# Windowed attention with two gated convolutions: turned probabilities in three blocks of 128 columns instead of four

## The chip, the cores and the metric

The program runs on one core of a Trainium2 chip. A core has TensorE (matmuls, PE in the profile, its weight loads PEld), VectorE (DVE), ScalarE (ACT), GpSimd (POOL) and SyncE (SP, which here issues all the DMAs). The metric is the device time of one execution in microseconds (us). The kernel before took 472.19 us, the median of three runs (470.36 to 472.33).

## The reference

The input is q, k and v of 4 batches, 8 heads, 576 positions, 64 per head. A query sees itself and the 127 keys before it, with a slope of its own for each head:

```
scores = q k^T / 8 ; mask = (0 <= i-j < 128)
scores = where(mask, scores - slope[h]*|i-j|, -1e9)
attn   = exp(scores - max) / (sum + 1e-9) ; x = attn v     # (4, 576, 512)
h = relu(x @ w_in)                                         # 512 -> 1024
conv_out = sum over 3 taps of conv_w[k] * h[s + k - 1]
x = (h * sigmoid(conv_out)) @ w_out                        # 1024 -> 512
gate = sigmoid(sum over 5 taps of conv_w2[k] * x[s + k - 4])
y = (gate * (x @ w_val)) @ w_out2                          # 512 -> 512
```

Everything is float32. The change touches only the product `attn v`.

## The kernel before, in words

**Attention in steps.** One step is one query tile `t` of 128 positions (five tiles to a sequence: 0 to 4, the last, `FULL`, has 64) and one pair of heads `hp`. There are 20 steps to a batch and 80 in all: 16 with t=0, 48 with t=1 to 3 (called full steps here), 16 with t=4. A tile is cut in two halves of 64 queries. The scores of one half are a matrix of 128 rows (64 queries of one head, then 64 of the other) by 192 keys: the queries of a half see the 128 keys before its first and its own 64. `scores` on PE (L732) makes them, DVE adds the bias and finds the maximum (L519), ACT takes the exponential and the sum (L388), DVE divides (L551).

**Turn and mix.** PE then turns the probabilities with the identity (`turn`, L746) so that keys lie on the partitions, ACT copies the turned ones from PSUM to `probs_t` (L399), and `mix` (L767) multiplies them with the values into `o_ps`. `probs` holds a half in 256 columns, of which 192 are used and 64 are zero, so that a block of 128 columns is always one whole key tile: a full step has two halves and two key tiles, so four blocks. `mix` goes over the key tiles `j`, the one before and the own one, and over the two heads; one matmul takes the 64 queries of both halves of that head, 128 columns, and its 64 output rows are the head's dimensions. So a full step has 4 matmuls of 128 columns, a step of t=0 has 2 of 128 columns (its own key tile alone), a step of t=4 has 4 of 64 columns (one half; its own key tile has 64 keys, so these matmuls use 64 rows of the array). The two heads write to different halves of the output partitions.

**A float32 matmul in the profile.** Turns have one record each; scores and mixes have two records for each matmul (288 matmuls of L767 and 576 records). "128*64" in a row is the part of the array in use: 128 rows (keys) by 64 columns (a head's dimensions).

**Products.** The four dense layers are `product` (L786 to L788): each block is three matmuls of 288 or 290 columns. They are worked in 8 chunks `c` of 288 positions, in 24 beats `j` each (`up`, `val`, `down`, `out`).

**The order.** It is written out by hand in `walk`. The first 12 steps run alone (`run`), the other 8 of the first batch run alone in the middle of chunk 0, and the other 60 stand one to a beat among the `down` products (12 matmuls to a beat): `slot` (turn of this step, scores three steps ahead), then the products of the beat, then `close`, the mix. Chunks 2, 4, 6 hold the 8 steps of t=3 and 4, chunks 1, 3, 5 the 12 of t=0 to 2. Engines meet at counting semaphores (`wait_ge`, `reach`): `probs_normal` (DVE has divided), `turned`, `copied` (ACT has copied), `mixed`.

## Time and profile before

| | |
|---|---|
| median of the runs | 472.19 us |
| time of the profiled execution | 472.24 us |
| its span (first to last instruction) | 470.5 us |
| PE busy, records | 444.9 us (95%), 3424 |
| PE weight loads busy | 413.7 us (88%) |
| DVE busy | 319.6 us (68%) |
| ACT busy | 283.0 us (60%) |
| mean granted clock of TensorE | 0.989 |

A row of a group of instructions names line, engine, operation, output and inputs, shapes and the number of records. PE records overlap, since matmuls are pipelined: how fast PE works is read from the distance of their starts, not from the mean duration. Of TensorE's clock, 1.00 is 2.4 GHz and 0.50 is 1.2 GHz.

### The profile page before, as it was taken

To read this page: it belongs to the slowest core of one execution; us is meant where nothing else is said; L and a number is where in the kernel's file an instruction comes from. 1 tells how busy PE (TensorE), PEld (TensorE's weight loads), DVE (VectorE), ACT (ScalarE), POOL (GpSimd) and SP (SyncE) were. 2 spreads that over 40 slices of the span, in tenths; PEclk is the share of its full clock that TensorE was granted. 3 is DMA by queue.
4 is the path that set the end of the run, shared out by engine and by line. 5 is a ranking of instruction groups with operands and counts; after the bars stand their busy time and mean duration, and the time that the engine had idled before them with its cause. 6 is when DMAs were issued, how large, how long until landed. Compare 5 with 4: busy or idle time off the path is not lost.

```text
span 470.5 us, 9646 instructions
## 1 busy us (share of the span) xinstructions
PE 444.9 (95%) x3424; PEld 413.7 (88%) x3424; DVE 319.6 (68%) x1128; ACT 283.0 (60%) x788; POOL 82.1 (17%) x116
## 2 busy tenths in 40 slices
PE   4888589988999999999999999999999999999996
PEld 3668559987999998999989999999989998899995
DVE  6695897866874777477675767757777576847741
ACT  3576942577556864497546874398555875287131
POOL 3210991071000410022000220013000230014000
PEclk9999869999999999999999999999999999999999
DMA  8765112001211012111211012011211100010011
GB/s 195 211 208 228 45 36 57 0 13 34 68 47 62 2 46 69 39 37 45 70 46 38 26 47 66 26 50 47 68 37 35 38 1 0 11 43 2 0 52 50
DMA packets 38927, 25.80 MB, mean 55 GB/s; under 512 B 22752, under 2 KB 35040, under 8 KB 38880
## 3 DMA queue, kind: packets, MB, share of 16 engines
q1 hardware_dynamic: 38880, 25.20, 18.7%
q8 instruction: 27, 0.44, 0.4%
q14 instruction: 20, 0.16, 0.1%
HBM read 20.47 MB, written 4.72 MB: 54 GB/s over the span
## 4 chain that ended last, share of the span: by engine, by line
PE 82%; DVE 7%; ACT 5%; issue 2%; DMA 1%; POOL 1%; SPq 1%; ACTq 0%; DVEq 0%
PE bank L786 20%; PE bank L787 20%; PE bank L788 20%; PE bank L732 8%; PE bank L767 7%; PE bank L746 7%; DMA k_all<-k_t 1%; DVE probs L551 1%; DVE probs L519 1%; ACT conv L426 1%; DVE w_lo L574 1%; DVE conv L604 1%; DVE gate L660 1%; ACT conv L432 1%; ACT bank L417 1%
## 5 line engine op out<-in xcount | busy, mean ns | idle before, releaser
L786 PE MATMUL bank<-g_hi,w_hi 128*128 128x288 f32 x384 | 120.8, 315 | 1.6 <-DVE g_lo L634 1.6
L786 PE MATMUL bank<-x_hi,w_hi 128*128 128x290 f32 (+1 forms) x384 | 114.5, 298 | 2.8 <-DVE x_lo L594 1.4
L787 PE MATMUL bank<-x_lo,w_hi 128*128 128x290 f32 (+1 forms) x384 | 114.0, 297 | 0.0
L788 PE MATMUL bank<-x_hi,w_lo 128*128 128x290 f32 (+1 forms) x384 | 113.7, 296 | 0.0
L787 PE MATMUL bank<-g_lo,w_hi 128*128 128x288 f32 x384 | 113.3, 295 | 0.0
L788 PE MATMUL bank<-g_hi,w_lo 128*128 128x288 f32 x384 | 113.3, 295 | 0.0
L357 POOL TENSOR_TENSOR g_lo<-conv,g_hi 128x288 fp32r<-128x288 f32 x64 | 51.9, 812 | 331.4 <-ACT g_hi L440 331.4
L604 DVE SCALAR_TENSOR_TENSOR conv<-bank,taps,conv 128x288 f32<-128x288 f32 (+1 forms) x128 | 65.5, 513 | 54.2 <-ACT conv L426 53.9
L388 ACT ACTIVATE probs<-probs,neg_max 128x192 f32<-128x192 f32 (+2 forms) x144 | 62.0, 432 | 33.1 <-DVE neg_max L519 31.6
L786 PEld LDWEIGHTS bank<-x_hi,w_hi 128*128 128x128 f32 x384 | 72.5, 189 | 3.5 <-DVE conv L612 1.8
L786 PEld LDWEIGHTS bank<-g_hi,w_hi 128*128 128x128 f32 x384 | 72.2, 188 | 2.6 <-issue 2.3
L788 PEld LDWEIGHTS bank<-x_hi,w_lo 128*128 128x128 f32 x384 | 72.7, 189 | 0.0
L787 PEld LDWEIGHTS bank<-x_lo,w_hi 128*128 128x128 f32 x384 | 72.5, 189 | 0.0
L787 PEld LDWEIGHTS bank<-g_lo,w_hi 128*128 128x128 f32 x384 | 72.2, 188 | 0.0
L788 PEld LDWEIGHTS bank<-g_hi,w_lo 128*128 128x128 f32 x384 | 72.2, 188 | 0.0
L399 ACT COPY probs_t<-bank 128x512 f32<-128x512 f32 (+1 forms) x80 | 39.9, 499 | 50.3 <-PE bank L746 49.8
L732 PE MATMUL bank<-k_all,q_tile 128*128 128x192 f32 (+2 forms) x288 | 61.5, 337 | 6.6 <-DMA k_all<-k_t 6.6
L660 DVE SCALAR_TENSOR_TENSOR gate<-bank,taps,gate 128x288 f32<-128x288 f32 (+4 forms) x128 | 65.3, 510 | 2.6
L746 PE MATMUL bank<-identity,probs 128*128 128x128 f32 x256 | 47.4, 300 | 9.2 <-DVE probs L551 9.0
L732 PEld LDWEIGHTS bank<-k_all,q_tile 128*128 128x128 f32 x288 | 47.3, 207 | 7.0 <-issue 5.7
L767 PE MATMUL bank<-probs_t,v_tile 128*64 128x128 f32 (+2 forms) x576 | 49.5, 284 | 2.7 <-ACT probs_t L399 1.4
L519 DVE CUSTOM_DVE_ANT_0 probs<-bank,bias 128x192 f32<-128x192 f32 (+2 forms) x144 | 46.2, 326 | 2.9 <-PE bank L732 2.5
(44 smaller groups left out, 519.0 us busy)
## 6 DMA issues: line engine op xcount, KB each, us to landing
w_raw<-panels SPq DMA_DIRECT2D x12, 512.0 KB, 6.1
y_t<-y_sb SPq DMA_DIRECT2D x32, 144.0 KB, 1.8
q_tile<-q_t SPq DMA_DIRECT2D x32, 128.0 KB, 3.1
k_all<-k_t SPq DMA_DIRECT2D x16, 256.0 KB, 3.6
v_tile<-v_tiles SPq DMA_DIRECT2D x16, 256.0 KB, 2.7
q_tile<-q_t SPq DMA_DIRECT2D x8, 64.0 KB, 2.4
k_all<-k_t SPq DMA_DIRECT2D x4, 128.0 KB, 2.7
v_tile<-v_tiles SPq DMA_DIRECT2D x4, 128.0 KB, 3.9
```

The source lines that it names most:

```text
L357: pool.tensor_tensor(g1_lo[:, m, :], conv[n % DEPTH][:, :], g1_hi[:, m, :], ALU.subtract).then_inc(g1_lo_done, 1)
L388: last = act.activation(probs[r][:, half, lo:hi], probs[r][:, half, lo:hi], ACT.Exp, bias=neg_max[r][:, half:half + 1], scale=-1.0, accum_ ...
L399: act.copy(probs_t[step % 2][:, 0:cols], t_ps[:, 0:cols]).then_inc(copied, 1)
L519: ins = dve.tensor_tensor_reduce(probs[r][:, half, lo:hi], s_ps[step % 2][:, 2 * P * half + lo:2 * P * half + hi], bias_of(hp, t, half), - ...
L604: dve.scalar_tensor_tensor(out=out, in0=banks[UP_BANK[m]][:, at + skip_first:at + HALF - skip_last], scalar=taps1[:, tap, m:m + 1], in1=ou ...
L660: dve.scalar_tensor_tensor(out=out, in0=banks[m][:, tap + skip:tap + HALF], scalar=taps2[:, tap, m:m + 1], in1=out, op0=ALU.mult, op1=ALU. ...
L732: last = pe.matmul(s_ps[step % 2][:, 2 * P * half + lo:2 * P * half + hi], q_tile[tile % 2][:, hp, half, :, :], k_all[:, hp, first_key + l ...
L746: last = pe.transpose(t_ps[:, at:at + P], probs[step % RING][:, half, col:col + P], identity[:, :])
L767: last = pe.matmul(o_ps[rows, P * hp:P * hp + SUB * subs], v_tile[key_tile % V_RING][0:keys, P * hp + HEAD * h:P * hp + HEAD * (h + 1)], t ...
L786: pe.matmul(out, w_hi[:, p, col:col + P], hi(k), start=start, stop=False)
L787: pe.matmul(out, w_hi[:, p, col:col + P], lo(k), start=False, stop=False)
L788: last = pe.matmul(out, w_lo[:, p, col:col + P], hi(k), start=False, stop=stop)
```

## The change

`probs` of a full step becomes 384 columns without a gap: half 0 in columns 0 to 191, half 1 in columns 192 to 383 (`packed`). Three blocks are turned instead of four (`blocks_of`). Block 0 is half 0 against the tile before, block 2 is half 1 against the own tile, and block 1 holds both rests: in its first 64 turned rows half 0 against the first 64 keys of the own tile, in its last 64 half 1 against the last 64 keys of the tile before. ACT copies 384 columns instead of 512. `mix` becomes up to four parts (`part`), each a pair of matmuls, one to a head, with the 64 queries of one half: own keys 0 to 63 (block 1), the tile before (block 0), own tile (block 2), keys 64 to 127 of the tile before (block 1). The last part first waits for the first (`upper_mixed`). A step of t=0 has the first and the third part and still two blocks; t=4 has the first and second part, with the same matmuls as before in another order. DVE clears 4 stretches of zeros at the start instead of 8.

```diff
--- before.py
+++ after.py
@@ -98,12 +98,12 @@
         v_tile = [place(f"v_tile{s}", [P, MODEL]) for s in range(V_RING)]
         bias = place("bias", [P, PAIRS, SEEN])
         identity = place("identity", [P, P])
-        probs = [place(f"probs{r}", [P, 2, 2 * P]) for r in range(RING)]
+        probs = [place(f"probs{r}", [P, 3 * P]) for r in range(RING)]
         neg_max = [place(f"neg_max{r}", [P, 2]) for r in range(RING)]
         total = [place(f"total{r}", [P, 2]) for r in range(RING)]
         guarded = [place(f"guarded{r}", [P, 2]) for r in range(RING)]
         inverse = [place(f"inverse{r}", [P, 2]) for r in range(RING)]
-        probs_t = [place(f"probs_t{r}", [P, 4 * P]) for r in range(2)]
+        probs_t = [place(f"probs_t{r}", [P, 3 * P]) for r in range(2)]
 
         g1_hi = place("g1_hi", [P, KW, HALF], F32R)
         g1_lo = place("g1_lo", [P, KW, HALF], F32R)
@@ -144,6 +144,7 @@
         turned = sem("turned")
         copied = sem("copied")
         mixed = sem("mixed")
+        upper_mixed = sem("upper_mixed")
         x_hi_done = sem("x_hi_done")
         x_lo_done = sem("x_lo_done")
         up_done = sem("up_done")
@@ -191,6 +192,16 @@
             lo, hi = columns_of(t, half)
             return bias[:, hp, lo - SUB * half:SEEN]
 
+        def packed(t, half):
+            lo, hi = columns_of(t, half)
+            return P * half + lo, P * half + hi
+        def blocks_of(t):
+            return {0: (1, 2), FULL: (0, 1)}.get(t, (0, 1, 2))
         def width_of(t):
             return TAIL if t == FULL else P
 
@@ -384,19 +395,19 @@
                 r = step % RING
                 act.wait_ge(scores_kept, step + 1)
                 for half in halves_of(t):
-                    lo, hi = columns_of(t, half)
-                    last = act.activation(probs[r][:, half, lo:hi], probs[r][:, half, lo:hi], ACT.Exp,
+                    lo, hi = packed(t, half)
+                    last = act.activation(probs[r][:, lo:hi], probs[r][:, lo:hi], ACT.Exp,
                                           bias=neg_max[r][:, half:half + 1], scale=-1.0,
                                           accum_out=total[r][:, half:half + 1])
                 last.then_inc(probs_done, 1)
 
             def slot(step):
                 _, t, _ = where(step)
-                cols = 2 * P if t in (0, FULL) else 4 * P
+                lo, hi = P * blocks_of(t)[0], P * blocks_of(t)[-1] + P
                 act.wait_ge(turned, step + 1)
 
                 reach(act, mixed, step - 1)
-                act.copy(probs_t[step % 2][:, 0:cols], t_ps[:, 0:cols]).then_inc(copied, 1)
+                act.copy(probs_t[step % 2][:, lo:hi], t_ps[:, lo:hi]).then_inc(copied, 1)
                 if step + LOOK - 1 < ALL_STEPS:
                     exps(step + LOOK - 1)
 
@@ -493,8 +504,7 @@
                 dve.memset(q_tile[s][HEAD:P, :, :, 0, :], 0.0).then_inc(q_zeroed, 1)
                 dve.memset(q_tile[s][0:HEAD, :, :, 1, :], 0.0).then_inc(q_zeroed, 1)
             for r in range(RING):
-                dve.memset(probs[r][:, 0, SEEN:2 * P], 0.0).then_inc(probs_zeroed, 1)
-                dve.memset(probs[r][:, 1, 0:SUB], 0.0).then_inc(probs_zeroed, 1)
+                dve.memset(probs[r][:, SEEN:2 * P], 0.0).then_inc(probs_zeroed, 1)
 
             def make_bias(hp):
                 for h in range(2):
@@ -515,9 +525,9 @@
 
                     reach(dve, turned, step - RING + 1)
                     dve.wait_ge(scores_done, step + 1)
-                lo, hi = columns_of(t, half)
+                (lo, hi), (to, end) = columns_of(t, half), packed(t, half)
                 ins = dve.tensor_tensor_reduce(
-                    probs[r][:, half, lo:hi], s_ps[step % 2][:, 2 * P * half + lo:2 * P * half + hi],
+                    probs[r][:, to:end], s_ps[step % 2][:, 2 * P * half + lo:2 * P * half + hi],
                     bias_of(hp, t, half), -SCALE, 3e38, ALU.add, ALU.min,
                     neg_max[r][:, half:half + 1])
                 if half == halves_of(t)[-1]:
@@ -547,8 +557,8 @@
                     return
                 if half == 0:
                     dve.wait_ge(inverse_done, step + 1)
-                lo, hi = columns_of(t, half)
-                ins = dve.tensor_scalar(probs[r][:, half, lo:hi], probs[r][:, half, lo:hi],
+                lo, hi = packed(t, half)
+                ins = dve.tensor_scalar(probs[r][:, lo:hi], probs[r][:, lo:hi],
                                         inverse[r][:, half:half + 1], None, ALU.mult)
                 if half == halves_of(t)[-1]:
                     ins.then_inc(probs_normal, 1)
@@ -738,13 +748,9 @@
                 _, t, _ = where(step)
                 pe.wait_ge(probs_normal, step + 1)
                 reach(pe, copied, step)
-                blocks = 1 if t == 0 else 2
-                for half in halves_of(t):
-                    for j in range(blocks):
-                        at = (blocks * half + j) * P
-                        col = (2 - blocks + j) * P
-                        last = pe.transpose(t_ps[:, at:at + P], probs[step % RING][:, half, col:col + P],
-                                            identity[:, :])
+                for n in blocks_of(t):
+                    last = pe.transpose(t_ps[:, P * n:P * n + P], probs[step % RING][:, P * n:P * n + P],
+                                        identity[:, :])
                 last.then_inc(turned, 1)
 
             def mix(step):
@@ -755,19 +761,32 @@
 
                     reach(pe, x_lo_done, tile)
                 pe.wait_ge(copied, step + 1)
-                blocks = 1 if t == 0 else 2
-                subs = len(halves_of(t))
-                turned_probs = probs_t[step % 2][:, 0:subs * blocks * P].rearrange(
-                    "p (a j h i) -> p a j h i", a=subs, j=blocks, h=2)
-                for j in range(blocks):
-                    key_tile = tile - blocks + 1 + j
-                    keys = width_of(t) if j == blocks - 1 else P
+                own, prev = v_tile[tile % V_RING], v_tile[(tile - 1) % V_RING]
+                def part(half, n, values, keys, start, stop):
                     for h in range(2):
-                        rows = slice(HEAD * h, HEAD * h + HEAD)
-                        last = pe.matmul(o_ps[rows, P * hp:P * hp + SUB * subs],
-                                         v_tile[key_tile % V_RING][0:keys, P * hp + HEAD * h:P * hp + HEAD * (h + 1)],
-                                         turned_probs[0:keys, :, j, h, :], start=(j == 0),
-                                         stop=(j == blocks - 1))
+                        at = P * hp + SUB * half
+                        heads = P * hp + HEAD * h
+                        last = pe.matmul(o_ps[HEAD * h:HEAD * h + HEAD, at:at + SUB],
+                                         values[keys, heads:heads + HEAD],
+                                         probs_t[step % 2][keys, P * n + SUB * h:P * n + SUB * h + SUB],
+                                         start=start, stop=stop)
+                    return last
+                reach(pe, mixed, step)
+                last = part(0, 1, own, slice(0, SUB), True, t == 0)
+                if 0 < t < FULL:
+                    last.then_inc(upper_mixed, 1)
+                if t > 0:
+                    last = part(0, 0, prev, slice(0, P), False, True)
+                if t < FULL:
+                    last = part(1, 2, own, slice(0, P), True, t == 0)
+                if 0 < t < FULL:
+                    pe.wait_ge(upper_mixed, step // STEPS * PAIRS * (FULL - 1) + step % STEPS - PAIRS + 1)
+                    last = part(1, 1, prev, slice(SUB, P), False, True)
                 last.then_inc(mixed, 1)
 
             def slot(step):
@@ -891,7 +910,7 @@
             for step in range(LOOK):
                 scores(step)
             pe.wait_ge(identity_made, 1)
-            pe.wait_ge(probs_zeroed, 2 * RING)
+            pe.wait_ge(probs_zeroed, RING)
             walk(slot, mix, beat)
 
 
```

On PE, a full step among the `down` products of chunk 1, before: the mix of the step, the turn and the scores of the next beat (v_tile_61 is the tile before, v_tile_59 the own one).

```order
L767 MATMUL bank<-probs_t_85,v_tile_61 64x128 [waits copied]
L767 MATMUL bank<-probs_t_85,v_tile_61 64x128
L767 MATMUL bank<-probs_t_85,v_tile_59 64x128 x2
L746 MATMUL bank<-identity,probs_66 128x128 [waits copied,probs_normal]
L746 MATMUL bank<-identity,probs_66 128x128 x3
L732 MATMUL bank<-k_all,q_tile_57 128x192 [waits scores_kept]
L732 MATMUL bank<-k_all,q_tile_57 128x192
```

The same place now. A row `64x64` is 64 output rows by 64 columns.

```order
L771 MATMUL bank<-probs_t_85,v_tile_59 64x64 [waits mixed,copied]
L771 MATMUL bank<-probs_t_85,v_tile_59 64x64
L771 MATMUL bank<-probs_t_85,v_tile_61 64x64 x2
L771 MATMUL bank<-probs_t_85,v_tile_59 64x64 x2
L771 MATMUL bank<-probs_t_85,v_tile_61 64x64 [waits upper_mixed]
L771 MATMUL bank<-probs_t_85,v_tile_61 64x64
L752 MATMUL bank<-identity,probs_66 128x128 [waits copied,probs_normal]
L752 MATMUL bank<-identity,probs_66 128x128 x2
L742 MATMUL bank<-k_all,q_tile_57 128x192 [waits scores_kept]
L742 MATMUL bank<-k_all,q_tile_57 128x192
```

Four matmuls of 128 columns have become eight of 64 in four parts, the first and the last on 64 keys; one turn of four has gone, and each mix waits for the mix before it and once for its own first part.

On PE, a step of t=0 in chunk 1, before:

```order
L767 MATMUL bank<-probs_t_84,v_tile_61 64x128 [waits copied,x_lo_done,v_loaded2]
L767 MATMUL bank<-probs_t_84,v_tile_61 64x128
L746 MATMUL bank<-identity,probs_65 128x128 [waits copied,probs_normal]
L746 MATMUL bank<-identity,probs_65 128x128
L732 MATMUL bank<-k_all,q_tile_56 128x192 [waits scores_kept,qk_loaded0]
L732 MATMUL bank<-k_all,q_tile_56 128x192
```

The same place now:

```order
L771 MATMUL bank<-probs_t_84,v_tile_61 64x64 [waits copied,mixed,x_lo_done,v_loaded2]
L771 MATMUL bank<-probs_t_84,v_tile_61 64x64 x3
L752 MATMUL bank<-identity,probs_65 128x128 [waits copied,probs_normal]
L752 MATMUL bank<-identity,probs_65 128x128
L742 MATMUL bank<-k_all,q_tile_56 128x192 [waits scores_kept,qk_loaded0]
L742 MATMUL bank<-k_all,q_tile_56 128x192
```

Two matmuls of 128 columns have become four of 64, of which the first two use 64 keys; the turns are as many as before.

## Rows read from the trace of the kernel before

**Rows 1.** Page, section 1: busy time, share of the span, instructions of each engine.
```profile
PE 444.9 (95%) x3424; PEld 413.7 (88%) x3424; DVE 319.6 (68%) x1128; ACT 283.0 (60%) x788; POOL 82.1 (17%) x116
```
**Rows 2.** Page, section 4: the chain that ended last, by engine.
```profile
PE 82%; DVE 7%; ACT 5%; issue 2%; DMA 1%; POOL 1%; SPq 1%; ACTq 0%; DVEq 0%
```
**Rows 3.** Stretches: length, busy time (records) of each engine, PE clock, DMA.
```profile
12.20:19.10 6.90, 6.90 (x29) 4.95 (x30) 4.00 (x18) 2.94 (x13) 2.34 (x4) 1.00 1.09 282
19.10:37.30 18.20, 15.28 (x132) 11.65 (x132) 16.89 (x78) 13.77 (x43) 2.37 (x4) 1.00 0.61 197
56.00:73.80 17.80, 14.22 (x104) 10.42 (x104) 17.23 (x57) 10.41 (x33) 15.53 (x20) 0.71 0.19 53
80.00:470.50 390.50, 383.12 (x2992) 362.35 (x2990) 257.98 (x894) 236.21 (x647) 49.36 (x62) 1.00 0.13 37
```
**Rows 4.** Waits of PE and PEld from 80 us: total us, times, longest.
```profile
PEld bank L767 <- issue: 11.3, 60, 1.6
...
PE bank L786 <- DVE g_lo L634: 1.6, 1, 1.6
PE bank L767 <- ACT probs_t L399: 1.4, 1, 1.4
PE bank L786 <- DVE conv L612: 1.3, 1, 1.3
```
**Rows 5.** PE in order of time, t=0: start, length, line, x records.
```profile
114.39 0.44 PE L767 MATMUL bank<-probs_t,v_tile 128*64 128x128 f32 x4
114.76 0.44 PE L746 MATMUL bank<-identity,probs 128*128 128x128 f32 x2
```
**Rows 6.** PE in order of time, full step among products.
```profile
120.57 0.66 PE L767 MATMUL bank<-probs_t,v_tile 128*64 128x128 f32 x8
121.16 0.66 PE L746 MATMUL bank<-identity,probs 128*128 128x128 f32 x4
121.65 0.82 PE L732 MATMUL bank<-k_all,q_tile 128*128 128x192 f32 x4
```
**Rows 7.** PE in order of time, two full mixes with nothing between.
```profile
35.55 1.09 PE L767 MATMUL bank<-probs_t,v_tile 128*64 128x128 f32 x16
```
**Rows 8.** PE in order of time, t=4 among products (the x8 are both forms).
```profile
182.79 0.60 PE L767 MATMUL bank<-probs_t,v_tile 128*64 128x64 f32 x8
183.31 0.44 PE L746 MATMUL bank<-identity,probs 128*128 128x128 f32 x2
183.59 0.33 PE L732 MATMUL bank<-k_all,q_tile 128*128 128x64 f32 x2
```
**Rows 9.** The same t=4 mix, its second form alone.
```profile
183.05 0.33 PE L767 MATMUL bank<-probs_t,v_tile 64*64 64x64 f32 x4
```
**Rows 10.** PE in order of time, two t=4 mixes with nothing between.
```profile
72.77 1.12 PE L767 MATMUL bank<-probs_t,v_tile 128*64 128x64 f32 x16
```
**Rows 11.** The t=4 mix cut at 182.79 and at 182.895 us: records begun till then.
```profile
182.79 0.27 PE L767 MATMUL bank<-probs_t,v_tile 128*64 128x64 f32 x1
...
182.79 0.33 PE L767 MATMUL bank<-probs_t,v_tile 128*64 128x64 f32 x3
```
**Rows 12.** Instructions of L767 from 80 us on: their count and forms.
```profile
L767 PE MATMUL bank<-probs_t,v_tile x432: 218/273/324, 108.4 to 408.0; 128*64 128x128 f32 x114, 128*64 128x64 f32 x15, 64*64 64x64 f32 x15
```
**Rows 13.** ACT's copies of turned probabilities: busy, mean ns, idle before.
```profile
L399 ACT COPY probs_t<-bank 128x512 f32<-128x512 f32 x48 | 28.1, 585 | 30.5 <-PE bank L746 30.1
L399 ACT COPY probs_t<-bank 128x256 f32<-128x256 f32 x32 | 11.8, 370 | 19.8 <-PE bank L746 19.7
```
**Rows 14.** Two pieces of the chain, first run of steps: start, length, what.
```profile
23.57 0.66 PE bank L746 x4
...
24.88 0.59 PE bank L767 x8
```
**Rows 15.** PE in order of time, second run of steps, clock at 0.50.
```profile
57.09 1.12 PE L746 MATMUL bank<-identity,probs 128*128 128x128 f32 x4 [4.86 <-DVE probs L551]
...
63.96 1.11 PE L746 MATMUL bank<-identity,probs 128*128 128x128 f32 x4 [0.27 <-DVE probs L551]
```


## The prediction

> **What bounds the kernel now.** I read the page's busy times and its chain of waits first, then the stretches, then the waits of PE, and last PE's instructions in order of time. PE is busy for 95% of the span and its weight loads for 88%, against 68% for the next engine [rows 1], and PE makes up 82% of the chain that ended last [rows 2]. The reader is to see that both say the same: what PE does is the time. The stretches say where this doesn't hold. From 80 us to the end PE is busy 383.12 of 390.50 us, while DVE has 258 and ACT 236 [rows 3], and PE's waits there for another engine come to 1.6 + 1.4 + 1.3 = 4.3 us [rows 4]. The 60 steps that stand among products lie in that part (432 records of L767 are 36 full steps of 8, 12 steps of t=0 of 4 and 12 of t=4 of 8 [rows 12]). In the first run of steps PE is busy 6.90 of 6.90 us while the steps of t=0 pass, and 15.28 of 18.20 us in the full ones; in the second run of steps it is DVE that has no room, 17.23 of 17.80 us, with PE at 14.22 [rows 3].
>
> **How PE's time in a mix is made up.** Record lengths mislead, since matmuls overlap; the distances of starts don't. Two full mixes with nothing between take 1.09 us as one group where one takes 0.66 [rows 6, 7], so eight more records cost 0.43 us. The two heads start together (three records have begun by 182.895 us, of which two are one pair [rows 11]), so this is four pairs of 128 columns at 0.11 us. A full mix runs from 120.57 to 121.16, 0.59 us [rows 6]: four pairs are 0.44, and 0.15 are left over. A mix of t=0, two pairs, runs from 114.39 to 114.76, 0.37 us [rows 5]: 0.22 and again 0.15. The rest doesn't grow with the pairs: it is the price of changing the part of the array in use (128*128 to 128*64 and back), once for each block of matmuls with one part. The row that decides is that of t=4. Its mix has two such blocks, 128*64 and then 64*64; the first begins at 182.79, the second at 183.05, the turn at 183.31 [rows 8, 9]. Each block takes 0.26 us for two pairs of 64 columns. Two mixes of t=4 back to back cost 1.12 against 0.60 [rows 8, 10]: 0.52 more for two more blocks. A pair of 64 columns is half of 0.11, 0.055, so each block is 0.11 for its pairs and 0.15 for the change. So a change of the rows alone, at the same 64 columns, costs as much as a change from 128*128. The Trainium skill says so too ("TensorEngine Tiling (Array Packing)", Tiling Modes, Key Properties: changing the tiling mode, not just the tile, drains TensorE); by that rule, and the trace agrees in the one direction it has, 128 rows to 64, the direction from 64 rows to 128 drains as well, which no row here shows.
>
> **The change part by part.**
>
> *Full step, mix.* Four parts: 64*64, then 128*64 twice, then 64*64. That is three blocks and eight pairs of 64 columns: 3 x 0.15 + 8 x 0.055 = 0.89 us against 0.59, so +0.30. The columns that pass through the array are the same as before; all that is added is two changes of the part in use. The change from 64*64 to 128*64 stands in no row. From below it is free, as the change within one form is [rows 7], from above it is the 0.15 of rows 8 and 9. I take 0.15, the nearest row: the same two forms, the other way round.
>
> *Full step, turn.* Four turns take 0.49 us (121.16 to 121.65 [rows 6]), two take 0.28 (183.31 to 183.59 [rows 8]): 0.11 for one that goes. Net +0.19 us for a full step. The Trainium skill gives some 0.275 us for a transpose of 128x128 in a kernel ("TensorE: Matmul & The Clock Gate", Part 4: PE-mode transpose). The trace has 0.11 at a granted clock of 1.00 and decides; by the page's figure the 36 full steps would gain 5.9 us more, an estimate of about 476 for the whole.
>
> *Step of t=0.* Two blocks and four pairs of 64: 0.30 + 0.22 = 0.52 against 0.37, +0.15. Turns as before. *Step of t=4.* The same two blocks in the other order: 0.
>
> *The new waits.* The fourth part waits for the first part's end. It could start 0.26 + 0.15 + 0.22 = 0.63 us after the first began; the first is over after 0.26 plus a tail: the last form's group reads 0.33 from 183.05 [rows 9]. So it is met 0.3 us early, and what is queued behind it (the last pair of parts, then the next turn) isn't held. The wait of a mix for the mix before is met a whole beat earlier. Taken at 0; were each to cost 0.05, it would be 36 x 0.05 = 1.8 us.
>
> *ACT's copy.* 512 columns take 585 ns, 256 take 370 [rows 13], so 384 take some 478, 0.11 less. Among products it was over long before the mix (PE waits once for it, 1.4 us [rows 4]): 0 there.
>
> *DVE.* The same instructions on the same columns, four clears fewer, which lie beside the first load. 0.
>
> **The sum.** From 80 us on, where PE has nothing to wait for, all of it is exposed: 36 x 0.19 = 6.8 and 12 x 0.15 = 1.8, 8.6 us. First run: three mixes of t=0 fall in the stretch in which PE is never idle, +0.45. Its eight full steps: if the old chain held, it has six turns of x4, two mixes of x8 and two copies (a turn and a mix of them in [rows 14]): 2 x 0.30 - 6 x 0.11 - 2 x 0.11 = -0.3. If PE's work set the pace, 8 x 0.19 = +1.5; PE has 2.9 us free there [rows 3]. I take +0.5. Second run: four full steps under DVE's cover (PE has 3.6 us free [rows 3]), I take +0.05, bounds -0.1 and +0.8. Sum 9.6 us. Against the profiled execution's own 472.24 us (span 470.5 and 1.7 around it) this gives 481.8. The median of the runs is 472.19, so it needs no shift.
>
> **Rivals.**
> 1. *The change from 64 rows to 128 is free.* Then a full step has two dear changes and gives +0.15 - 0.11 = +0.04, t=0 gives 0: 36 x 0.04 = 1.5 us and nothing at the start, 473.9, no change to be measured. For it: no row shows this direction. Against it: the other one costs 0.15, and so do the ones to and from 128*128.
> 2. *Faster: rows can be changed without a stop when the 64 columns stay.* The place is inside each mix, and the price -0.11 us for each full step: 36 x -0.11 = -4.0, with -0.3 in the first run, 467.9. It decides from the point where such a change costs less than 36 x 0.11 / (2 x 36 + 12) = 0.047 us. Against it stands 182.79 to 183.05 for two pairs that need 0.11 [rows 8, 9].
> 3. *It is the number of records that costs.* The t=4 mix has 0.53 us for 8 records, 0.066 each; if that were a rate of issue, 16 records would take 1.06 and a full step +0.47 - 0.11 = +0.36: 36 x 0.36 + 12 x 0.16 + about 1.6 at the start is 16.5, 488.7. Against it: three records have begun within 0.11 us [rows 11], and 128-column records pass at 0.43 / 8 = 0.054 [rows 6, 7]. For it: nowhere do more than four records of 64 columns follow each other in one form. The Trainium skill has such a rate, some 62 ns for each MATMUL when the sequencer decodes in microcode ("TensorE: Matmul & The Clock Gate", Part 2: What happens when you issue a matmul); the row of 0.054 lies under it.
> 4. *The clock falls in the first run of steps.* It fell to 0.50 around 56 us, after PE had been idle for 4.86 us [rows 15]; the first run has no such gap, but its mixes get emptier. Cold steps take (63.96 - 57.09) / 2 = 3.4 us [rows 15] against 18.2 / 8 = 2.3 [rows 3]: some +9, 491.
>
> **How the numbers follow.** Forecast 0.79, rival 1 0.05, rival 2 0.05, rival 3 0.08, rival 4 0.03. The forecast's own range is 479 to 484.5: below, the first run at its lower bound and part of the row change hidden; above, the new waits at 0.05 each and the first run fully exposed. The range given, 478.5 to 489, takes in rival 3 and leaves out 1, 2, 4 and some tails, under 2 in 10. A change of 0.5%, 2.4 us, is about what can be told from none. Slower by over that: 0.79 + 0.08 + 0.03, less 0.01 for a forecast that fails in part, 0.89; within it 0.05; faster 0.06.
>
> **What would show it.** In the profile after, a full mix among products should run from its first start to the next turn in 0.89 us, with three blocks: 64*64 of 4 records (0.26), 128*64 of 8 (0.37), 64*64 of 4 (0.26). The full turn should go from 0.49 to 0.38, the mix of t=0 from 0.37 to 0.52, the beat of a full step grows by 0.19. The copies should read some 478 ns, the weight loads of L767's successor should show more idle time put down to issue than the 11.3 us of 60 times [rows 4], and the stretch of the second run should be as long as before. If the middle block starts within 0.15 us of the first, rival 1 or 2 is right; if the four pairs of the middle block take more than 0.25 us between their starts, rival 3. A row in which the fourth part waits for the first would show that the new wait isn't hidden.

## The result, and the profile after

The changed kernel takes 487.38 us, the median of four runs (485.66 to 490.24), against 471.27 before: a ratio of 1.0345 (95% interval 1.0311 to 1.0379), so 16 us slower. The forecast was 481.8 in a range of 478.5 to 489.0, chance of slower 0.89. The direction and, for the 60 steps among products, the mechanism were right, the size was not: 9.6 us forecast, some 16 measured. The profiled execution took 490.24 us, span 488.5, and is the slowest of the four; its lengths are read here, and the whole by the ratios. Medians below are of all runs of a kernel, while the ratios leave out three runs that lie over 1.5% above their kernel's fastest: one of 848.95 us in experiment 2, and 492.64 and 491.92 us in experiment 4.

From the page after: busy time, share and records of the engines, and the granted clock of TensorE in 40 slices, as in [rows 1].

```profile
PE 466.2 (95%) x3824; PEld 432.5 (89%) x3824; DVE 318.7 (65%) x1124; ACT 277.5 (57%) x788; POOL 82.3 (17%) x116
...
PEclk9998955999999999999999999999999999999999
...
PE 84%; DVE 5%; ACT 5%; issue 2%; DMA 1%; POOL 1%; SPq 1%; ACTq 0%; DVEq 0%
```

PE has 21 us more of busy time and is as full as before. What differs is the granted clock: in the sixth and seventh slice, 61 to 86 us, it is at 0.50, its lower level of 1.2 GHz, where before it was there for some 10 us, and the 8 in the fourth slice is a shorter low stretch (mean over the span 0.972, before 0.989).

PE among the products in the changed kernel, in order of time: start, length, group, records. First a step of t=0, then a full one; a group carries the form of its first record. They answer to [rows 5] and [rows 6].

```profile
124.31 0.60 PE L771 MATMUL bank<-probs_t,v_tile 64*64 64x64 f32 x8
124.84 0.33 PE L752 MATMUL bank<-identity,probs 128*128 128x128 f32 x1
...
134.32 0.97 PE L771 MATMUL bank<-probs_t,v_tile 64*64 64x64 f32 x16
135.22 0.55 PE L752 MATMUL bank<-identity,probs 128*128 128x128 f32 x3
135.60 0.33 PE L742 MATMUL bank<-k_all,q_tile 128*128 128x192 f32 x1
```

The mix of t=0 runs from 124.31 to 124.84, 0.53 us (forecast 0.52, before 0.37). The full mix runs from 134.32 to 135.22, 0.90 us (forecast 0.89, before 0.59), in blocks of 0.26, 0.38 and 0.26 by the starts of its single records, and the turn from 135.22 to 135.60, 0.38 (forecast 0.38, before 0.49). The rest of what was forecast is there too: ACT's copies, and PE's waits from 80 us on, which answer to [rows 13] and [rows 4].

```profile
L410 ACT COPY probs_t<-bank 128x384 f32<-128x384 f32 x48 | 23.0, 479 | 36.3 <-PE bank L752 36.1
```

```profile
PEld bank L771 <- issue: 12.0, 62, 1.7
...
PE bank L805 <- DVE g_lo L644: 1.6, 1, 1.6
PE bank L771 <- ACT probs_t L410: 1.5, 1, 1.5
PE bank L805 <- DVE conv L622: 1.3, 1, 1.3
...
PE bank L771 <- PE bank L771: 0.2, 1, 0.2
```

The last of these rows is one group of records, the last mix of the second run of steps:

```profile
81.08 0.89 PE L771 MATMUL bank<-probs_t,v_tile 64*64 64x64 f32 x8 [0.16 <-PE bank L771]
```

A copy takes 479 ns, and PE waits for other engines as little as before. The 0.16 us is a mix of t=4, which has no fourth part: it waits for the mix just before it, and the same happens where the last two mixes of the first run follow each other. The wait of a mix's fourth part for its first stands in no row, so it is hidden. One sign that was named hardly came: the idle of the weight loads put down to issue is 12.0 us here after 11.3. The new pauses inside a mix are hardly listed as waits; they are seen in the distances of starts.

What was not forecast is the first batch. Stretches of the changed kernel: length, busy time (records) of PE, PEld, DVE, ACT, POOL, then the clock. They are the first run of steps, the first products behind it, the second run, the first products behind that, and from the first mix among products to the last.

```profile
12.00:38.00 26.00, 25.15 (x204) 19.35 (x204) 19.09 (x89) 14.68 (x52) 5.03 (x8) 1.00 0.64 188
...
41.00:44.30 3.30, 3.01 (x12) 3.01 (x13) 0.24 (x1) 0.00 (x0) 0.00 (x0) 0.50 0.99 375
...
61.70:82.00 20.30, 19.58 (x134) 14.53 (x134) 16.10 (x57) 9.01 (x33) 14.14 (x18) 0.50 0.16 40
...
82.00:85.30 3.30, 3.30 (x14) 3.30 (x15) 0.42 (x1) 0.37 (x1) 0.00 (x0) 0.50 0.27 79
...
118.00:428.00 310.00, 309.71 (x2683) 289.41 (x2684) 205.59 (x770) 188.43 (x539) 32.72 (x41) 1.00 0.14 38
```

In the second run it was DVE that had no room, 17.23 of 17.80 us, with PE at 14.22 [rows 3]. Now PE has 19.58 of 20.30 and DVE 16.10: the bound has changed hands. The 18.0 us between the two profiled executions can be laid out by the starts of PE's instructions:

| stretch | before | now | more |
|---|---|---|---|
| start to the first product | 38.1 us | 41.3 us | 3.2 |
| from there to the first turn behind it | 12.9 | 14.6 | 1.6 |
| that turn to the next one (PE mostly waits for DVE) | 6.1 | 5.9 | -0.2 |
| the second run from there, to the first product behind it | 16.7 | 20.2 | 3.4 |
| from there to the first mix among products | 34.5 | 36.2 | 1.6 |
| to the end | 362.1 | 370.4 | 8.3 |

The last line is the one that the forecast had. The two of 1.6 us are the products that pass at the low clock, and the 3.4 lie in the second run. The first line is in part chance. Four records of the same scores, at the start and later, in the changed kernel and then in the one before:

```profile
17.65 1.49 PE L742 MATMUL bank<-k_all,q_tile 128*128 128x192 f32 x4
...
25.83 0.82 PE L742 MATMUL bank<-k_all,q_tile 128*128 128x192 f32 x4
```

```profile
14.89 1.49 PE L732 MATMUL bank<-k_all,q_tile 128*128 128x192 f32 x4
...
21.12 0.82 PE L732 MATMUL bank<-k_all,q_tile 128*128 128x192 f32 x4
```

At the start they follow each other at 0.32 us, later at 0.16, though the column of the granted clock reads 1.00 for both. The change comes at 23.9 us in the changed kernel's profile and at 18.4 in the one before; in the fourteen profiles of this case it lies between 13.1 and 23.9 us. The same changed kernel profiled again (experiment 3) has it at 19.7 and its first product 2.2 us earlier.

### The profile page after: what moved, and what is told of

Its sections match the earlier page's. It is cut to its first block, busy times and chain, and to the rows that moved or that the text cites. A ratio compares the mean times of both kernels' runs of the same rounds, so it can differ in the third digit from the quotient of the medians.

```text
span 488.5 us, 10521 instructions
## 1 busy us (share of the span) xinstructions
PE 466.2 (95%) x3824; PEld 432.5 (89%) x3824; DVE 318.7 (65%) x1124; ACT 277.5 (57%) x788; POOL 82.3 (17%) x116
## 4 chain that ended last, share of the span: by engine, by line
PE 84%; DVE 5%; ACT 5%; issue 2%; DMA 1%; POOL 1%; SPq 1%; ACTq 0%; DVEq 0%
PE bank L805 19%; PE bank L806 19%; PE bank L807 19%; PE bank L771 12%; PE bank L742 8%; PE bank L752 6%; DMA k_all<-k_t 1%; ACT conv L437 1%; DVE probs L561 1%; DVE probs L529 1%; DVE conv L614 1%; DVE gate L670 1%; ACT conv L443 1%; ACT bank L428 1%; ACT g_hi L451 1%
## 5 line engine op out<-in xcount | busy, mean ns | idle before, releaser
L771 PEld LDWEIGHTS bank<-probs_t,v_tile 128*64 128x64 f32 (+1 forms) x1024 | 49.5, 142 | 27.9 <-issue 16.0
L771 PE MATMUL bank<-probs_t,v_tile 128*64 128x64 f32 (+1 forms) x1024 | 70.4, 252 | 2.4 <-ACT probs_t L410 1.5
L742 PE MATMUL bank<-k_all,q_tile 128*128 128x192 f32 (+2 forms) x288 | 64.3, 348 | 6.4 <-DMA k_all<-k_t 6.4
L410 ACT COPY probs_t<-bank 128x384 f32<-128x384 f32 (+1 forms) x80 | 34.9, 436 | 60.2 <-PE bank L752 60.0
L742 PEld LDWEIGHTS bank<-k_all,q_tile 128*128 128x128 f32 x288 | 49.7, 217 | 6.9 <-issue 5.5
L752 PE MATMUL bank<-identity,probs 128*128 128x128 f32 x208 | 43.5, 314 | 6.3 <-DVE probs L561 6.0
```

The source lines that it names most:

```text
L410: act.copy(probs_t[step % 2][:, lo:hi], t_ps[:, lo:hi]).then_inc(copied, 1)
L742: last = pe.matmul(s_ps[step % 2][:, 2 * P * half + lo:2 * P * half + hi], q_tile[tile % 2][:, hp, half, :, :], k_all[:, hp, first_key + l ...
L752: last = pe.transpose(t_ps[:, P * n:P * n + P], probs[step % RING][:, P * n:P * n + P], identity[:, :])
L771: last = pe.matmul(o_ps[HEAD * h:HEAD * h + HEAD, at:at + SUB], values[keys, heads:heads + HEAD], probs_t[step % 2][keys, P * n + SUB * h: ...
```

## Experiments

Each kernel ran beside the kernel before, on one chip within a group; "us" is the median, the ratio that to the kernel before.

**1. All parts on 128 rows.**

```diff
-last = part(0, 1, own, slice(0, SUB), True, t == 0)
+last = part(0, 1, own, slice(0, SUB if t == FULL else P), True, t == 0)
-last = part(1, 1, prev, slice(SUB, P), False, True)
+last = part(1, 1, prev, slice(0, P), False, True)
```

> The changed kernel, in which the parts on 64 keys use all 128 rows of the array (steps of t=0 to 3; t=4 keeps its 64). It so adds the rows of the other half, so this leaves the masking of block 1 out of the computation. Same number of matmuls, records, columns, turns and waits as in the changed kernel. Theory A (a change of the part of the array in use costs 0.15 us): the mix of a full step falls from 0.90 to 0.15 + 8 x 0.055 = 0.59, that of t=0 from 0.53 to 0.37, and with three turns instead of four the kernel is 4 us faster than the one before, 467 to 468, if TensorE's clock comes back to the mean of 0.989. Rival B (the number of records costs): the full mix stays at 0.85 to 0.90 and the time at 485 or more. Theory C, on the clock: if the low clock of the first batch comes from the emptier array, it is back with this one (mean over 0.985); if it comes from the missing turns, it stays near 0.972 and the time is 472 to 475.

This kernel leaves out the masking of block 1, so what it computes is not this attention, and it is of use for its time alone. Measured: 472.28 us against 472.14, ratio 1.0001 (0.9978 to 1.0024). PE in order of time, a full step:

```profile
124.58 0.74 PE L771 MATMUL bank<-probs_t,v_tile 128*64 128x64 f32 x16
125.25 0.55 PE L752 MATMUL bank<-identity,probs 128*128 128x128 f32 x3
```

The same 16 records take 0.67 us instead of 0.90, so it isn't their number that costs (rival 3, theory B), and about 16 us by the ratios are gone with the rows alone. It isn't 0.59 as expected, either: 0.08 too much. In the single records, 0.05 of it is a pause at the fourth part: its weight load starts 0.06 after the last matmul of the third part has started, where the others start at once, and it is the only one with a wait. So with the pauses of the row changes gone, the wait for the first part, whose cover they were, comes into sight; the prediction had put it at nothing, and in the changed kernel that holds. The rest is pairs at 0.058 instead of 0.054. A full step is then 0.08 - 0.11 = -0.03 us against before, and the kernel is level where 467 to 468 us were expected. The clock's mean was 0.985, nearly back, with three turns as in the changed kernel, so the missing turn isn't what keeps it low. Whether that is the fewer rows in use or the pauses at their changes, this kernel takes both away and doesn't tell.

**2. The new form in the first batch alone, and in the rest alone.** The two forms side by side in one kernel, chosen by the step (two lines of the edit; the other kernel has `step >= STEPS`):

```diff
+def new_form(step):
+    return step < STEPS
```

> The new form in the 20 steps of the first batch alone, the old one in the other 60. It measures the first batch alone. If what the forecast missed (16 us measured, 9.6 forecast, with 9.2 of it among products) is the first batch with its lower clock, this kernel is 6 to 8 us slower than the one before, 477 to 479, with the mean clock near 0.972. If the first batch is only dearer by its own mode changes (forecast 1.0 us), it is at 472 to 473. The zeros are put back by four small clears at the change of form, under 0.5 us of VectorE.

> The other way round: the old form in the first batch, the new one in the 60 steps among products. By the forecast's term (36 x 0.19 + 12 x 0.15 = 8.6; with the starts read from the new trace 9.2 and 0.9 of it given back at the ends of chunks) it is 8 to 9.5 us slower than before, 479.5 to 481, with the mean clock at 0.989 as before. If the clock's fall is tied to the mixes among products it shows here too, and the time is over 483.

Measured: first batch alone 479.46, ratio 1.0139 (1.0093 to 1.0186), mean clock 0.971; rest alone 480.83, ratio 1.0175 (1.0140 to 1.0211), mean clock 0.989. Against 472.14, by the medians, that is +7.3 and +8.7, and the sum of 16.0 is the whole difference. By the ratios it is 6.6 (4.4 to 8.8) and 8.3 (6.6 to 10.0), 14.8 of 16.3, which is the whole within the intervals. The 60 steps among products cost what the forecast said (8.6). The 20 steps of the first batch cost some seven times what it said (1.0). Of the four runs of the second kernel one took 848.95 us at a mean clock of 1.00; why isn't known.

**3. Inside the first batch: first run alone, second run alone, and the changed kernel again beside them.**

```diff
+    return step < FIRST
```

```diff
+    return FIRST <= step < STEPS
```

> The new form in the first 12 steps alone (8 full, 4 of t=0), where PE has 2.9 us free. If the mode changes alone cost there: +0.5 to +2 us, ratio 1.001 to 1.004, clock 0.989. If it is this run that lowers the clock behind it (a low stretch around 40 us, as in the changed kernel and in the one with the new form in the first batch): +4 to +6 us, ratio 1.009 to 1.013.

> The new form in steps 12 to 19 alone (4 full ones, 4 of t=4 that differ in order alone). By the forecast VectorE covers all of it: 0 to +0.8 us, ratio 1.000 to 1.002. If the emptier mixes keep the clock low until the products are back (23.9 us in the changed kernel against 10.2 before), PE becomes the bound of this run: +3 to +5 us, ratio 1.006 to 1.011, and the low stretch is over 17 us here too.

> The changed kernel itself once more, beside the next three on one chip: 485 to 489 and a mean clock of 0.970 to 0.976, with low stretches again near the end of the first run (some 41 us) and through the whole second run. If the clock is 0.985 or more in this profile and the time lies under 484, the clock's share was chance.

Measured, beside 471.07 before: first run 474.04, ratio 1.0063 (1.0034 to 1.0092); second run 476.00, ratio 1.0086 (1.0050 to 1.0121), 4.1 us by the ratio and 4.9 by the medians; the changed kernel 488.86, ratio 1.0356 (1.0318 to 1.0395), mean clock 0.968. The profile of the one with the second run alone, that run:

```profile
56.00:76.30 20.30, 19.58 (x134) 14.54 (x134) 16.24 (x60) 9.05 (x33) 14.15 (x18) 0.50 0.16 40
```

PE's busy time and the length repeat those of the changed kernel's row to the hundredth: the low clock and the length of 20.3 us come from the new form in these very steps (four full ones; in those of t=4 only the order differs), and not from what ran before. In the first run of steps the granted clock reads 1.00 until its end; the profile of the one with that run alone then shows 0.91 over the stretch behind it, among the first products:

```profile
19.10:36.00 16.90, 15.51 (x178) 11.99 (x177) 15.71 (x73) 11.30 (x39) 2.89 (x4) 1.00 0.67 205
36.00:56.00 20.00, 15.76 (x104) 15.46 (x104) 11.69 (x26) 13.92 (x34) 8.00 (x12) 0.91 0.31 112
```

Its 3.0 us are between the two cases expected. They can be divided by estimate. From the first product to the first turn behind it took 14.5 us here and 12.9 before, so the low stretch behind the run costs 1.6. It appears in five of the seven profiles that have the new form in the first run (in those with more turns and with the filled idle, below, a stretch of the same length stands at 110 and 115 us instead), and in none of the other seven. The steps' own price is some 0.7 us, from the one pair of profiles that reach the faster pace at about the same time (experiment 2: 17.9 and 18.1 us): the first product starts at 38.43 us with the new form in the first run and at 37.77 with the old.

**4. What holds the clock: more work for PE in the second run, as turns or as matmuls.** Into 128 unused columns, ahead of the turn in each of the 8 steps:

```diff
+for _ in range(4):
+    pe.transpose(t_ps[:, 3 * P:4 * P], identity[:, :], identity[:, :])
```

```diff
+for _ in range(2):
+    pe.matmul(t_ps[:, 3 * P:4 * P], identity[:, :], identity[:, :], start=True, stop=True)
```

> The changed kernel with four more turns (of the identity, into unused columns of the PSUM bank) ahead of the turn in each of the 8 steps of the second run, 0.44 us of PE a step at full clock. It pairs with the next kernel. What is asked: what brought the clock back at 66 us in the kernel before and left it low until 85 us in the changed one. Theory C1 (any busy PE counts): both fillers shorten the low stretch of 23.9 us to 17 or less. Theory C2 (turns count less than matmuls): only the next one does. Theory C3 (it is the idle before the run and chance of when the chip looks): neither does. PE has some 5 us free in this run, so the filler itself costs 0 to 2 us.

> The same with two float32 matmuls of 128 columns on 128 x 128 instead of the four turns: also 0.44 us of PE a step at full clock. C1: as the one with turns; C2: the low stretch falls to 17 us or less and the time by 1 to 3 us here alone; C3: as the changed kernel, 487 to 488, plus up to 2.

Measured, beside 472.03: with turns 486.36, ratio 1.0271 (1.0225 to 1.0318); with matmuls 485.54, ratio 1.0267 (1.0224 to 1.0310). Both have work added and are not slower than the changed kernel (1.0345 and 1.0356 on other chips); they look some 0.8% faster, but the intervals meet or all but meet, on different chips and with one run of each kernel left out, so that is likely and not shown. The profile of the one with turns, in the second run: mixes before and after the clock's return.

```profile
58.89 1.51 PE L774 MATMUL bank<-probs_t,v_tile 64*64 64x64 f32 x16
...
62.66 0.98 PE L774 MATMUL bank<-probs_t,v_tile 64*64 64x64 f32 x16
...
64.81 0.97 PE L774 MATMUL bank<-probs_t,v_tile 64*64 64x64 f32 x16
66.85 0.97 PE L774 MATMUL bank<-probs_t,v_tile 64*64 64x64 f32 x16
```

Here the clock returned around 63 us, in the midst of the run, and a full mix fell from 1.51 to 0.97. In the changed kernel it stayed low to the end of the run. The profile of the one with matmuls is of its run of 491.92 us, and its low stretch lasts from 61 to 78 us, while its second run of steps ends at 84.8:

```profile
61.00:78.00 17.00, 15.17 (x99) 12.12 (x99) 12.91 (x33) 6.95 (x21) 15.79 (x21) 0.50 0.09 23
```

So the low stretch of the second run is some 7 and 17 us long with the fillers. In the five profiles that have the new form there without filler in the steps (that of experiment 5 is one of them) it is 20 to 27 us long, in the other seven 10 to 14, in experiment 1 in two pieces. The mean clock of every run says the same: 0.989, 0.982, 0.968 and 0.989 with turns, 0.976, 0.989, 0.986 and 0.989 with matmuls, against 0.968 to 0.975 in all ten runs of the changed kernel. Turns worked as well as matmuls, so C2 falls. C3 as it was put, that neither does, falls too; but with two of the eight runs near the old clock and 7 against 17 us, chance has a part in it.

**5. The idle ahead of the second run filled.**

```diff
+if step == FIRST:
+    for _ in range(20):
+        pe.matmul(t_ps[:, 3 * P:4 * P], identity[:, :], identity[:, :], start=True, stop=True)
```

> The changed kernel with 20 float32 matmuls of 128 columns (into unused columns of PSUM) in the 4.75 us in which PE waits for the first turn of the second run: 20 x 0.21 = 4.3 us of matmuls in place of the idle. If the idle is what lowers the clock there, the clock is at 1.00 from there until the products, the second run is 16 to 18 us long instead of 20, and the kernel 3 to 5 us faster than the changed one, 482.5 to 484.5. If the clock falls all the same for the steps' own sake, the time is 486 to 488.

Measured: 488.13, ratio 1.0350 (1.0315 to 1.0386): no gain. The filler stretch, the run behind it, and that run's third turn:

```profile
51.60:56.10 4.50, 4.50 (x42) 4.50 (x41) 3.63 (x9) 3.54 (x10) 4.21 (x8) 1.00 0.00 0
56.10:78.50 22.40, 19.52 (x143) 14.61 (x141) 17.86 (x61) 10.81 (x36) 15.76 (x20) 0.61 0.24 60
```

```profile
61.67 0.90 PE L752 MATMUL bank<-identity,probs 128*128 128x128 f32 x3 [2.08 <-DVE probs L561]
```

The idle was gone and the clock at 1.00 when the run began, and it fell to 0.50 at 60.9 us, within the run, all the same, and stayed there until 81.3. The idle of 4.9 us [rows 15] isn't what keeps it low, then. What the steps do alone isn't quite shown for the fall itself: PE stood idle for 2.08 us in the run when it came. For the 20 us after it, with PE busy nearly all the time, it is the steps that don't bring it back. The second of the two cases expected, 486 to 488, is the one that came.

**6. The price of a change of rows, alone.** The kernel before with t=4 on 128 rows:

```diff
-keys = width_of(t) if j == blocks - 1 else P
+keys = P
```

> The kernel before with one edit: the matmuls of t=4 on its own key tile use 128 rows instead of 64 (the turned probabilities of the other 64 rows are zero, so the result is the same). It takes one change of the part in use out of each of the 16 mixes of t=4 and touches nothing else: same records, columns and waits. Theory A: the mix of t=4 falls from 0.527 to 0.37 us and the kernel by 12 x 0.155 = 1.9 us, 470.3 against 472.1 (ratio 0.996), the four of the first batch being covered by VectorE. Rival: if the 0.15 us belongs to the change of key tile and not to that of the rows, the mix stays at 0.53 and the ratio at 1.000.

Measured: 470.31 against 472.03, ratio 0.9953 (0.9932 to 0.9974). PE, a step of t=4:

```profile
186.46 0.45 PE L767 MATMUL bank<-probs_t,v_tile 128*64 128x64 f32 x8
186.84 0.44 PE L746 MATMUL bank<-identity,probs 128*128 128x128 f32 x2
```

0.38 instead of 0.52 us [rows 8], 0.14 to 0.15 for the one change taken away, and the rival named, the change of key tile, falls. It is the cleanest test of the theory: records, columns and waits are the same, and the kernel before gets faster by using twice the rows.

**7. Three turns without the new parts.** ScalarE puts the halves of block 1 in two places, and the mix is the old one. The copies of a full step:

```diff
+act.copy(to[:, :].rearrange("p (a c) -> p a c", a=4)[:, 0:4:3, :],
+         t_ps[:, 0:4 * P].rearrange("p (a c) -> p a c", a=4)[:, 0:3:2, :])
+act.copy(to[SUB:P, P:2 * P], t_ps[SUB:P, P:2 * P])
+act.copy(to[0:SUB, 2 * P:3 * P], t_ps[0:SUB, P:2 * P]).then_inc(copied, 1)
```

> Three turns as in the changed kernel, but ScalarE copies the halves of block 1 to two places of a probs_t of four blocks whose other halves stay zero, and the mix is the old one: 2 or 4 matmuls of 128 columns on 128 rows. A full step has three copies instead of one: 256 columns 0.37 us and two of 64 partitions by 128 columns, estimated at 0.26 each from the two sizes in the rows (0.585 at 512, 0.370 at 256), 0.89 instead of 0.585 in all. Theory A: among products 36 x -0.11 = -4.0 us, no new mode change, copies hidden beside the products; the first run of steps has the copy on its chain twice (+0.6) and six turns less (-0.65). 467 to 468.5. If the longer copy delays the mixes it shows as waits of PE's L-line of the mix for ACT, and the gain is under 2 us.

> Padded copies with the mixes as before, and t=4 on 128 rows as well: the candidate for the fastest. If the two gains add, 467.0 - 1.9 = 465.1, ratio 0.985 (0.982 to 0.988).

Measured: 466.98 against 472.14, ratio 0.9887 (0.9851 to 0.9923); with t=4 on 128 rows 466.36 against 472.03, ratio 0.9869 (0.9839 to 0.9900), which ends nearer to the first than the sum of both gains, but within the intervals. ACT's copies in the first of them, and PE in a full step:

```profile
L420 ACT COPY probs_t<-bank 64x128 f32<-64x128 f32 x80 | 20.7, 259 | 0.5
L417 ACT COPY probs_t<-bank 128x256 f32<-128x256 f32 x48 | 17.8, 370 | 20.2 <-PE bank L765 19.7
L419 ACT COPY probs_t<-bank 64x128 f32<-64x128 f32 x48 | 12.5, 260 | 0.6
```

```profile
126.06 0.66 PE L785 MATMUL bank<-probs_t,v_tile 128*64 128x128 f32 x8
126.64 0.55 PE L765 MATMUL bank<-identity,probs 128*128 128x128 f32 x3
```

The mix is at 0.58 to 0.59, and the turn has three records. The copies take 0.89 us in all, as estimated, and cost nothing beside the products. By the ratio the kernel gains 5.3 us, where 4.0 were forecast for the turns among products and 3.6 to 5.1 expected for the whole. So the saved turn is worth at least what the forecast said; it was the price paid for it on PE that was too high. The second of the two is the fastest of all kernels run here.

## Why the prediction was right, and where it was short

*The bound, and what a mix is made of.* Right: blocks at 0.15 us and pairs at 0.055 gave 0.89, 0.52 and 0.38; measured 0.90, 0.53 and 0.38. The unseen change from 64 rows to 128 costs as much as the seen one. Experiments 1 and 6 show from two sides that it is the rows and not the records, which takes rivals 1 to 3 away.

*The 60 steps among products.* Right: 8.6 forecast, 8.7 measured alone (experiment 2).

*The new waits.* Right for this kernel, by a cover that the prediction named only in part: experiment 1 shows 0.05 us for the wait as soon as the pauses around it are gone. The wait for the mix before is not met everywhere: it costs 0.16 us at the end of each run of steps, where two mixes follow each other.

*The first batch.* Here the term of the sum was mis-sized: +1.0 forecast (0.45 + 0.5 + 0.05), +7.3 measured alone by the medians, 6.6 by the ratio. Of it the first run has 3.0 us by its ratio, where the two terms came to 0.95 with 1.95 as the upper bound; the steps themselves are some 0.7 of it by the estimate of experiment 3, which is near the forecast, and the rest is the low clock behind them. The second run has 4.1 us by its ratio (1.0086), where 0.05 was taken and 0.8 was the bound. The step that failed is "four full steps under DVE's cover (PE has 3.6 us free)". The free time was read as fixed, but it held only at the clock that this stretch happened to have: 0.71 over it [rows 3]. With the new mixes the clock stayed at 0.50, all of PE's work in the run grew, DVE's cover was used up and PE became the bound; the products behind the run then passed at the low clock too. Rival 4 had the fall of the clock, with a chance of 0.03, but put it in the first run. It came just behind that run, for 3.4 us, and above all in the second, where the clock was low for a part already [rows 15], and the new steps didn't bring it back. Its price there, 4 to 5 us with the products behind it, is about half of the 9 named.

*Readings that were off.* The term of 0.45 for three mixes of t=0 takes their length at the full clock, but in that stretch PE's records run at half pace under a granted clock that reads 1.00 [rows 3], and each mix grew by 0.19 (0.63 to 0.82), not 0.15. A turn's record is 0.27 to 0.33 us long while turns follow each other at 0.11; so the 0.275 that the prediction set beside its 0.11 is like the length of a record and is no second price. Rival 1 adds up to 473.7, not 473.9.

*The range* held the result by luck: it reached up to rival 3, which was not the reason. The forecast's own range, 479 to 484.5, didn't hold it.

## What to carry to other kernels

Count the blocks of matmuls that use one part of the array, in rows as well as in columns: here each block cost 0.15 us, more than a turn of 128 columns (0.11), so half the rows with zeros in them were cheaper than a change to half the rows. Where a cost is called covered by another engine, work out the cover again at the lower clock if the stretch's clock isn't 1.00, and count the work behind the stretch that would pass at it too. And before saving work on the bound engine by splitting other work on it, see whether an idle engine can do the splitting: three copies on ScalarE did it for nothing.

## What the runs showed of the hardware that was not expected

- In the second run PE was busy for 19.58 of 20.30 us by the profile and its clock stayed at 0.50 throughout; with four turns a step added it returned midway (one profile, and a mean clock of 0.982 or more in three of four runs), and with 20 matmuls ahead of the run it fell nonetheless. A busy PE in the profile is not enough to have the full clock.
- From the start until 13.1 to 23.9 us, in all fourteen profiles, PE's records of 192 columns followed each other at 0.32 us and from then on at 0.16, and the column of the granted clock read 1.00 throughout. A stretch at the start has to be checked by the distances of starts.
- A change of 128 rows to 64 or back at the same 64 columns costs 0.15 us, as one from 128*128 to 128*64 does.
- In experiment 1 PE's wait for its own earlier matmul cost 0.05 us with no pause to cover it: that matmul's record had begun 0.24 us before the point where the next weight load would have started, and 0.29 before it did.
